# Wider moving operands for the narrow products of an attention stage, and one read moved behind a turn

## The reference

```
attention (B,H,S,Ns,D = 8,8,512,32,64), scale = 1/sqrt(D)
  a  = softmax(scale * x @ state^T);   xread = a @ state     # 512 rows per batch and head
  a2 = softmax(scale * state @ x^T);   sread = a2 @ x        # 32 "slot" rows
  rows = concat(xread, sread), heads side by side            # 4352 rows of 512
mixture of experts (E = 8, F = 1024)
  logits = rows @ w_gate;  e = argmax;  p = softmax(logits)[e]
  g = sigmoid(rows @ w_output_gate)[e]
  rows = p * g * (relu(rows @ w1[e]) @ w2[e])                # only the chosen expert
dense layer (2048 wide)
  h = rows @ w_in;  out = gate(h) @ w_out
  gate(h) = h for h >= 1, 0 for h <= -1, (h + 1)^2 / 4 between
```

## Time and profile before

| | us |
|---|---|
| median of three runs | 1383.74 |
| the three runs | 1394.68, 1383.74, 1382.07 |
| the profiled execution | 1402.41 |
| its span, first to last instruction | 1400.7 |

### The profile page before, as it was taken

One profiled execution on the slowest core, in us unless ns is written; L12 is line 12 of the kernel. 1 busy time (PEld: TensorE's weight loads), 2 busy tenths in 40 slices (PEclk: granted clock), 3 DMA queues, 4 the chain that ended last, 5 costly groups with the idle time before them and its releaser, 6 DMA issues.

```text
span 1400.7 us, 19926 instructions
## 1 busy us (share of the span) xinstructions
PE 1361.7 (97%) x6621; PEld 1145.0 (82%) x6622; DVE 800.6 (57%) x1512; ACT 406.5 (29%) x640; POOL 386.7 (28%) x213
## 2 busy tenths in 40 slices
PE   6999989999999999999999999999999999999996
PEld 6998878888888888878888888888888888888885
DVE  3568768888888877883444444444444444444343
ACT  2344322222222223232222222222222222222232
POOL 2246545177566256944010010100101001000010
PEclk9989889999999999999999999999999999999998
DMA  7344524143435143442010010100100001000000
GB/s 196 74 123 138 154 98 165 45 165 125 144 108 170 54 156 105 165 120 85 20 42 15 15 38 16 38 15 15 38 15 29 23 15 37 15 12 27 0 31 16
DMA packets 80442, 100.28 MB, mean 72 GB/s; under 512 B 46096, under 2 KB 46096, under 8 KB 79888
## 3 DMA queue, kind: packets, MB, share of 16 engines
q1 hardware_dynamic: 62128, 62.21, 14.6%
q10 hardware_dynamic: 11744, 19.67, 4.5%
q0 software_dynamic: 6528, 17.87, 3.4%
HBM read 69.80 MB, written 29.92 MB: 71 GB/s over the span
## 4 chain that ended last, share of the span: by engine, by line
PE 92%; DVE 3%; issue 1%; DMA 1%; SPq 1%; ACT 0%; another core or an unknown queue 0%; POOLq 0%; ACTq 0%; DVEq 0%; POOL 0%
PE area L1535 27%; PE area L1549 26%; PE area L1467 15%; PE area L1481 14%; PE area L1294 2%; PE area L1266 2%; PE area L1285 2%; PE area L1441 1%; PE area L1521 1%; DVE record_now L907 1%; PE area L1311 1%; PE area L1366 1%; PE area L1259 1%; DMA xin<-in_x 0%; DMA yrow<-sorted_y 0%
## 5 line engine op out<-in xcount | busy, mean ns | idle before, releaser
L1549 PE MATMUL area<-W,gs 128*128 128x512 f32 x1632 | 397.7, 392 | 1.0 <-DVE gs L1176 1.0
L1535 PE MATMUL area<-ys,W 128*128 128x512 f32 (+1 forms) x1728 | 394.4, 377 | 0.0
L1535 PEld LDWEIGHTS area<-ys,W 128*128 128x128 f32 x1728 | 313.4, 188 | 61.2
L1549 PEld LDWEIGHTS area<-W,gs 128*128 128x128 f32 x1632 | 303.0, 188 | 63.1 <-DVE gs L1176 1.4
L1123 DVE STREAM_TRANSPOSE area<-hrow 32x256 f32<-32x256 f32 x592 | 269.8, 456 | 79.6 <-ACT hrow L691 70.7
L754 ACT ACTIVATE gate<-gate,half_col 128x512 f32<-128x512 f32 (+1 forms) x144 | 100.7, 700 | 441.0 <-DVE gate L1171 439.8
L598 POOL DMA_INDIRECT out<-orow,out_row x34 | 32.8, 963 | 708.6 <-ACT orow L770 619.0
L1171 DVE TENSOR_SCALAR gate<-area 128x512 f32<-128x512 f32 (+1 forms) x144 | 95.3, 662 | 224.6 <-PE area L1535 224.5
L1481 PE MATMUL area<-W,hs 128*128 x912 | 217.5, 394 | 0.0
L1467 PE MATMUL area<-W,xs 128*128 x888 | 209.7, 392 | 4.4 <-issue 4.4
L1467 PEld LDWEIGHTS area<-W,xs 128*128 128x128 f32 x888 | 167.5, 189 | 39.7 <-issue 4.8
(11 more groups left out here) (175 smaller groups left out, 863.0 us busy)
## 6 DMA issues: line engine op xcount, KB each, us to landing
stage<-in_moe_w SPq DMA_DIRECT2D x32, 1024.0 KB, 5.5
sorted_y<-ytile ACTq DMA_DIRECT2D x38, 256.0 KB
xtile<-slot_x ACTq DMA_DIRECT2D x36, 256.0 KB
yrow<-sorted_y SPq DMA_DIRECT2D x34, 256.0 KB, 2.6
xin<-in_x SPq DMA_DIRECT2D x64, 128.0 KB, 2.9
stage<-in_moe_w_in SPq DMA_DIRECT2D x4, 1024.0 KB, 5.0
stage<-in_moe_w_out SPq DMA_DIRECT2D x4, 1024.0 KB, 7.1
slot_x<-zero SPq DMA_DIRECT2D x8, 256.0 KB, 3.1
```

The lines of the kernel that those rows point to most:

```text
L1535: last = nc.tensor.matmul(HIDDEN[n % 2][:, 0:width], wq[:, wp, :], ys[par][:, yp, k, 0:width], start=(k == 0 and wp == HI and yp == HI), s ...
L1549: last = nc.tensor.matmul(SUMS[a], gs[n % 2][:, gp, a * P:(a + 1) * P], W[:, q // 2 + 2, wp, at:at + DM], start=(n == 0 and gp == HI and w ...
```

## The change

Five groups of products stream more columns of their moving operand; what they compute beyond the old result is overwritten by the next product or read by nobody.

- `scores`: for the first three pairs of heads, 128 columns instead of 64; the 64 added are the neighbouring entry in `stT`, and what they give lies where the next pair's scores are then written.
- `slots_rows`: likewise 128 instead of 64 for three pairs, the next pair's columns of `p2`.
- `gates_of_slots`: the 16 gate columns four times over (64 columns); the copy of VectorE takes the first 16 of each 64.
- The slots' logits and the last batch's logits: the 16 columns eight times over (128); the copies take the first 16 of each 128.
- At the seam `read_rows(r, 3)` with its wait on `xread_copied[1]` moves from ahead of `turn_p2(1)` to behind it.

```diff
+    G4 = 4 * G
+    G8 = 8 * G
-        LAST_LOGITS = bank(0)[:, 0:CH * G]
-        SLOT_LOGITS = bank(1)[:, 0:ST * 2 * E]
+        LAST_LOGITS = bank(0)[:, 0:CH * G8]
+        SLOT_LOGITS = bank(1)[:, 0:ST * G8]
...
-                                             pC[:, 0:B * 2 * G].rearrange("p (b g e) -> p b g e", g=2, e=G)[:, :, g, :])
+                                             pC[:, 0:B * 2 * G4].rearrange("p (b g e) -> p b g e", g=2, e=G4)[:, :, g, 0:G])
...
+            def over(v, times):
+
+                return v.unsqueeze(1).to_broadcast([P, times, G])
...
-                        last = nc.tensor.matmul(pC[2 * NS * q:2 * NS * (q + 1), n * 2 * E:(n + 1) * 2 * E],
-                                                stT[:, q, n, :], gate_w[:, j, :, :].rearrange("p n e -> p (n e)"),
+                        last = nc.tensor.matmul(pC[2 * NS * q:2 * NS * (q + 1), n * G4:(n + 1) * G4],
+                                                stT[:, q, n, :], over(gate_w[:, j, :, :].rearrange("p n e -> p (n e)"), 4),
                                                 start=True, stop=True)
...
+            def pairs_wide(j):
+
+                return 2 if j < PAIRS - 1 else 1
+
             def scores(s, j):
+                wide = pairs_wide(j)
+                states = stT[:, :, :, :].rearrange("p q i n -> p (q i) n")
                 for c in range(CH):
                     at = c * HN + j * 2 * NS
-                    last = nc.tensor.matmul(pA[:, at:at + 2 * NS], xT[:, j, c * P:(c + 1) * P],
-                                            stT[:, j % 2, bass.ds(2 * s + j // 2, 1), :].rearrange("p o n -> p (o n)"),
+                    last = nc.tensor.matmul(pA[:, at:at + wide * 2 * NS], xT[:, j, c * P:(c + 1) * P],
+                                            states[:, bass.ds(2 * s + (j % 2 * (B * PAIRS // 2) + j // 2), wide), :
+                                                   ].rearrange("p o n -> p (o n)"),
                                             start=True, stop=True)
...
+                    wide = pairs_wide(j)
                     for c in range(CH):
-                        last = nc.tensor.matmul(pC[:, j * 2 * NS:(j + 1) * 2 * NS], xin[other][:, c, 2 * j:2 * j + 2, :],
-                                                p2[:, c, j * 2 * NS:(j + 1) * 2 * NS],
+                        last = nc.tensor.matmul(pC[:, j * 2 * NS:(j + wide) * 2 * NS], xin[other][:, c, 2 * j:2 * j + 2, :],
+                                                p2[:, c, j * 2 * NS:(j + wide) * 2 * NS],
                                                 start=(c == 0), stop=(c == CH - 1))
...
-            pe.wait_ge(xread_copied[1], 2 * r + 1)
-            read_rows(r, 3)
             pe.wait_ge(prob2_done, b + 1)
             pe.wait_ge(xread_copied[0], 2 * r + 2)
             turn_p2(1)
+            pe.wait_ge(xread_copied[1], 2 * r + 1)
+            read_rows(r, 3)
             pe.wait_ge(p2_copied, b + 1)
...
-                    last = nc.tensor.matmul(SLOT_LOGITS[:, t * 2 * E:(t + 1) * 2 * E], sT[:, k, t * P:(t + 1) * P],
-                                            gate_w[:, k, :, :].rearrange("p n e -> p (n e)"),
+                    last = nc.tensor.matmul(SLOT_LOGITS[:, t * G8:(t + 1) * G8], sT[:, k, t * P:(t + 1) * P],
+                                            over(gate_w[:, k, :, :].rearrange("p n e -> p (n e)"), 8),
...
-                    last = nc.tensor.matmul(LAST_LOGITS[:, c * G:(c + 1) * G], pT[:, g, c * P:(c + 1) * P],
-                                            st_diag[:, b, at:at + G], start=(g == 0), stop=(g == 1))
+                    last = nc.tensor.matmul(LAST_LOGITS[:, c * G8:(c + 1) * G8], pT[:, g, c * P:(c + 1) * P],
+                                            over(st_diag[:, b, at:at + G], 8), start=(g == 0), stop=(g == 1))
```

More of the change, by code:

```diff
@@ L994, in _ @@
             dve.wait_ge(slogit_made, 1)
-            nc.vector.tensor_copy(record_now[0][:, 0:ST, 0:2 * E], SLOT_LOGITS.rearrange("p (t e) -> p t e", t=ST)
+            nc.vector.tensor_copy(record_now[0][:, 0:ST, 0:2 * E], SLOT_LOGITS.rearrange("p (t e) -> p t e", t=ST)[:, :, 0:G]
                                   ).then_inc(logit_copied, 1)
@@ L998, in _ @@
             dve.wait_ge(logit_made, 1)
-            nc.vector.tensor_copy(record_now[1][:, :, 0:G], LAST_LOGITS.rearrange("p (c e) -> p c e", c=CH)
+            nc.vector.tensor_copy(record_now[1][:, :, 0:G], LAST_LOGITS.rearrange("p (c e) -> p c e", c=CH)[:, :, 0:G]
                                   ).then_inc(logit_copied, 1)
```

## The result

The changed kernel takes 1382.83 us (median of 20 runs, 1379.2 to 1387.78). The kernel before was run 20 times as well, and its median is now 1391.97 us (1382.07 to 1395.33), not the 1383.74 of the first three. The ratio is 0.9945, with a 95% interval of 0.9927 to 0.9962: 0.55% faster; the medians lie 9.1 us apart. The time is inside the stated range, by 0.2 us, but the gain is less than half of those 21 us.

The account below looks back on a forecast made before the run. TensorE was taken as the bound, with gains only in the first 210 us, where its clock falls. Start 7, steps 7, seam 8, moved read 0.3, less 1 for width: 21 us, 1402.4 to 1381, less 10 gives 1371; range 1361 to 1383.

Parts of the forecast that it names:

- those 21 us: Whole kernel: the forecast gain, 7 + 7 + 8 + 0.3 - 1 us, taken off the profiled 1402.4 us.
- the width: Scores, slot rows and logits: 416 instructions widened to 128 columns cost 1 us in sum, at most 20.
- Rival (C): Widened products: added columns come on top of weight loads, 20 us; 1391 with the clock won, 1404 without; chance 0.08.
- Start: Steps 0 and 1: the clock rises during step 0's scores rather than at 44 us; about 7 us won, bounds 0 and 9.
- The gate products of the slots: Step 0, 64 instructions going from 16 to 64 columns: 0 taken, range 0 to 2 us loss.
- Steps 2 and 3: The first clock fall of the steps, 3.4 us long, goes: 1.7 us won.
- Steps 4 to 7: 77.2 us with 17 at half clock become about 72, the wait behind VectorE's addition remaining: 5.2 us won, bounds 2 and 8.5.
- Seam: 165.30 to 184.58 us: slot rows, turns, logits and reads at full clock; 8 us won, bounds 0 and 8.5.
- the moved read: At the seam: the read covers the copy of p2, with 0.9 us idle ahead of the turn; 0.3 us won, bounds -0.6 and +1.0.
- From the profiled execution to the median: Of the 18.7 us between them, 8.5 taken as clock and 10 as the profiler's own: 1381 - 10 = 1371 us.
- The reading of the clock: TensorE: under narrow products the clock stays low or falls at a short stall, and wide ones bring it back.
- Rival (B): Clock falls remain or VectorE keeps the gain; only 4 to 8 us of start and seam won, 1378 us; chance 0.27.

Follow-up runs that it names:

- run 20: Not a label but a count: the unchanged kernel before was run 20 times, median 1391.97 us (1382.07 to 1395.33).
- the kernels with the split cut: GpSimd's low-part split of the first expert's weights made for 64 of 2048 columns: on the changed kernel 1376.44 us, on the kernel before (narrow) 1377.97 us.
- the executions of the table: Seven profiled executions of kernels with narrow or wide scores, cut at the same places into stages; their starts take 41.6 to 51.4 us.
- the three other narrow ones: Changed kernel with scores and slot rows narrow (1387.8 us); kernel before with the split cut (1377.97) or held behind the expert choice, two scatters behind the division (1380.19).
- the kernel with 16-column logits: The kernel before with scores and slot rows alone widened, gate products and logits as before, read at the seam not moved: 1384.61 us.
- the version that beats both: Changed kernel, split held behind the expert choice, two scatters behind the division, third expert-weight unit loaded behind x for batch 5: 1373.16 us, ratio 0.9864.

## Why the prediction was right and wrong

**What bounds the kernel, and the width: right.** The gain is all ahead of the experts, and 128 columns take nearly the time of 64. The whole price was put at 1 us. The rows give 0.3 us a step where TensorE is the bound, 2.5 us at most in eight steps. Rival (C) is out: in steps 2 and 3 wide and narrow are both 31.3 us in the kernels with the split cut. If the columns came on top of the weight loads, 128 would be slower than 16, and at full clock 16 instructions take 1.79 us with 128 columns and 1.8 us with 16. That the flat time goes with the weight load, these traces show in two places: with 16 moving columns at half clock an instruction takes 213 ns with 128 stationary columns and 3.60/64 = 56 ns with 64, and at full clock the weight loads of 16 instructions take 1.86 us both for 16 columns (slot logits, scores and slot rows alone wide) and for 128 (slot rows after).

**Start: right.** 7 forecast, 7.0 measured. The clock record begins at 16.5 us instead of 44.4, the 44 us of the forecast, and shows one fall in the idle stretch named beforehand, 6.8 us long where 3.4 were allowed for (26.8 to 33.6). That the clock was at half ahead of 44.4 us is read from durations (score instructions of 210 ns in steps 0 and 1, 110 ns in step 2); the record doesn't show it. The gate products of the slots, put at 0 to 2 us, take 2.08 us from 21.50 us with 64 columns, and TensorE idles 1.80 us behind them: no loss. In the executions of the table the starts with narrow and wide scores are 2.4 to 9.8 us apart.

**Steps 2 and 3: right for this pair of executions.** 1.7 forecast, 2.1 measured. The fall that was won back is in the profiled execution before alone; the three other narrow ones take 31.0 to 31.4 us.

**Steps 4 to 7: wrong in the profiled execution, and the largest error of mechanism.** "Four steps at about 18 us: 72, so 5.2 us are won" became 76.9 us, 0.1 won. The step of the argument that failed is that the wait for `onehot` would stay what it was in step 7. I had the mechanism in hand (the addition runs long while GpSimd splits) and took its length from one step. In this execution the addition starts with GpSimd's division instead of near its end: 6.2 to 6.7 us instead of 5.0, a stall of 2 us instead of 1.25, and behind three of the four stalls 3.4 us at half clock, 1.7 us lost each time. In them products of 128 columns run, which the prediction had named as a sign against it. Stalls 8.2 us and falls 5 us are 13 us, against 11.3 us between the profiles of the changed kernel and the one with the split cut. The forecast is nearly met where the addition keeps its old place: 72.7 us in the execution with scores and slot rows alone wide. In the one with the read not moved the additions take 5.8 to 6.6 us, one fall follows and the steps take 74.1 us. So the wait varies from one execution to the next, and the sum had one value for it. Why the addition comes when it does in each, no run shows.

**Seam: the size met by luck.** 8.3 forecast with the moved read, 7.8 measured. The wide logits were not needed for it, as the kernel with 16-column logits shows, and the narrow kernels of the table with 21.7 and 23.6 us show that most of the 7.8 is a stretch at half clock of the one profiled execution before. The moved read shifted the idle time as worked out, 1.15 us ahead of the turn (0.9 forecast) and 0.18 ahead of the slot rows (from 1.10), but won nothing: from the first count to the first slot-row product it is 3.50 us (152.63 to 156.13), and 3.48 before (161.82 to 165.30). In the prediction's working 165.3 - 164.9 is 0.4 and not 0.3, and its seam, 165.30 to 184.58, is 19.3 us and not 19.1; neither matters.

```profile
153.94 1.09 PE L1317 MATMUL area<-ident,prob2T 128*128 128x128 f32 x8 [1.15 <-DVE prob2T L957]
154.87 1.08 PE L1298 MATMUL area<-st_diag,pT 128*128 128x272 f32 x4
156.13 1.05 PE L1308 MATMUL area<-p,xin 128*128 128x128 f32 x7 [0.18 <-ACT p L668]
```

**The rest: a term I left out.** The prediction says of the stretch behind 210 us that it "has nothing that could vary". It varies. Behind the seam the changed kernel's execution is 2.3 us longer. At the passage from experts to the dense layer TensorE waits for a store and a load of rows in turn, 2.85 us at 585 us here and 1.75 before, and here a fall of the clock follows (586.5 to 589.9). Over the twelve experiments and both kernels this last stretch ran from 1208 to 1213 us in no relation to the edit. The five executions with a fall of the clock at this passage are the five longest (1210.9 to 1212.5 us; the others 1208.4 to 1210.6). That is noise of 4 us that the profile of one execution can't average.

**From the profiled execution to the median: wrong, and the main reason that 1371 was too low.** "I take 8.5 and 10", the 10 being the profiler's own. Nothing of the sort exists in these numbers: over the changed kernel and the twelve experiments the profiled execution lies from 4.9 us below to 6.3 us above the median of its kernel, 0.7 us above it on average. The execution before was simply a bad one (of the 78 later runs of that kernel beside the experiments two were slower, the worst 1405.46), and the median of the first three a lucky one, 8 us below that of 20. Without that subtraction the sum reads 1402 - 21 = 1381, close to the measured 1382.83, but by luck. Terms read from this one execution (the 17 us at the seam, the fall of step 3) stand for more than the usual execution has to give: from 1392 to 1383 the medians differ by 9 us, not 21.

**The reading of the clock: half right.** I held that narrow products lose the clock and wide ones keep it. At the start it holds in all executions of the table: up to the end of the start the clock is low, or not yet up, for 18 to 23 us with wide scores and for 33 to 44 us with narrow ones. Later it is less clear: stalls of 2 us cost the wide kernel its clock too, and with the stalls away the medians of narrow and wide are 1.5 to 4.4 us apart instead of 9. Rival (B), with 0.27, is nearest to what happened: falls remain, and in the profiled execution VectorE kept the gain of the steps. The time of 1378 that it gave was 5 us low, from the same wrong baseline.

## What to carry to other kernels

When a resource comes back (here the clock), the wait that was hidden under the slow stretch doesn't only appear, it can grow (here from 1.25 us to 1.8 to 2.3), when the engines arrive at another moment of their neighbour's work: bound such a collision by the longest overlap that the order allows, not by the row you have. In this kernel the small VectorE addition with two operands in SBUF, on the critical path, belonged at a point where GpSimd doesn't run its split (0.22 to 0.40 us in steps 4 to 7 with the split and half of the scatters moved, 6.2 to 6.7 in those of the changed kernel), and a semaphore that holds back the split cost less than the collision (medians 1375.75 and 1382.83 us). And take the median of many executions before working out a difference of one per cent: three runs put this baseline 8 us wrong, and one profile showed falls of the clock that other executions don't have.

## What the runs showed of the hardware that I had not expected

- A VectorE operation of 4 elements a partition took 3.49 us, and one of 64 took 6.48, against 0.17 and 0.22 us clear of GpSimd's long operations (in the version that beats both), each ending within 0.1 us of the end of GpSimd's split.
- The record of the granted clock begins with its first rise, and what lies ahead of it is counted as full speed: before, the window from 13 to 22 us shows 1.00, and the 32 score instructions in it take 6.73 us against 3.52 in step 2. The profiled execution before, whose record begins at 44 us, shows a mean of 0.983 and took 1402.41 us; seven other executions of the kernel with 0.983 took 1383.82 to 1402.14 us. Means can't be compared without looking at the start.
- The same stall doesn't always cost the clock. At the seam, behind 1.10 us of idle time, 64-column slot rows ran into a fall in the kernel before and kept full clock in the narrow kernel with the split cut; 128-column ones kept it in the run without the moved read. Stalls of 1.8 to 2.3 us took it from wide products in three cases of four in the changed kernel, and in one of two (2.03 and 2.19 us) in the run without the moved read.
